# Where the on-chip buffers of a two-stage FFN kernel lie: declared in another order, so that operands and tiles start at multiples of 128 bytes

## What is computed

```python
w = softmax(weight, axis=-1)                       # 8 heads x 7 taps
x = einsum('hk,bskhg->bshg', w, windows(x_pad))    # 7 taps along the sequence
gate = 1 / (1 + exp(-(x @ moe_w_gate)))            # 192 -> 1536
y = (gate * (x @ moe_w_val)) @ moe_w_out           # 1536 -> 192
h = y @ moe2_w_in                                  # 192 -> 2048
g = where(h > 0, h, exp(min(h, 0)) - 1)
out = g @ moe2_w_out                               # 2048 -> 192
```

## Time and profile before

| What | Value |
|---|---|
| Median of 3 runs | 1220.97 us (1220.84 to 1221.13) |
| The profiled execution, its own time | 1221.01 us |
| Its span, first to last instruction | 1219.2 us |
| PE busy | 1203.1 us, 99% of the span |
| Weight loads (PEld) busy | 1147.8 us, 94% |
| DVE busy | 922.2 us, 76% |
| ACT busy | 631.1 us, 52% |
| POOL busy | 89.3 us, 7% |

### The profile page before, as it was taken

The page is one execution under the profiler, slowest core; times in us unless marked ns, Lnnn a source line. Parts: engine busy times, 40 slices in busy tenths (PEclk is TensorE's granted clock), DMA queues, the critical chain, the costliest instruction groups (busy, mean ns, idle before and its releaser), DMA issues.

```text
span 1219.2 us, 27136 instructions
## 1 busy us (share of the span) xinstructions
PE 1203.1 (99%) x10220; PEld 1147.8 (94%) x10220; DVE 922.2 (76%) x1497; ACT 631.1 (52%) x1093; POOL 89.3 (7%) x87
## 2 busy tenths in 40 slices
PE   5999999999999999999999999999999999999998
PEld 4998888888899999999999999999999999999998
DVE  7788777787777877778777777777777777777786
ACT  6555445454554545545455453544535555455554
POOL 4271001010010100001010010100101001010000
PEclk9999999999999999999999999999999999999999
DMA  6021101001010010100101001110101101001000
GB/s 203 22 68 36 31 18 34 30 17 30 17 34 30 17 30 17 47 17 17 30 25 40 17 17 30 35 30 17 30 19 33 30 17 34 30 17 30 10 10 26
DMA packets 14022, 38.04 MB, mean 31 GB/s; under 512 B 2224, under 2 KB 2224, under 8 KB 14000
## 3 DMA queue, kind: packets, MB, share of 16 engines
q1 hardware_dynamic: 13776, 37.60, 10.7%
q10 hardware_dynamic: 224, 0.14, 0.0%
HBM read 15.71 MB, written 6.29 MB: 18 GB/s over the span
## 4 chain that ended last, share of the span: by engine, by line
PE 98%; DVE 1%; ACT 1%; DMA 0%; issue 0%; SPq 0%; DVEq 0%; ACTq 0%
PE hid L236 55%; PE z_acc_a L254 14%; PE y_acc_a L254 11%; PE z_acc_b L254 10%; PE y_acc_b L254 8%; DMA raw_g<-g_weights 0%; DVE mixed L646 0%; ACT gw L470 0%; PE y_acc_a L236 0%; DVE h_split L673 0%; ACT L526 0%; ACT curve L482 0%; SPq L173 0%; ACT ys L604 0%; ACT ys L599 0%
## 5 line engine op out<-in xcount | busy, mean ns | idle before, releaser
L236 PE MATMUL hid<-xs,gw 64*128 64x512 f32 x3240 | 621.1, 393 | 0.0
L236 PEld LDWEIGHTS hid<-xs,gw 64*128 64x128 f32 x3240 | 507.4, 185 | 17.3
L236 PE MATMUL hid<-ys,ew 64*128 64x512 f32 x2160 | 471.2, 393 | 0.0
L487 ACT CAST h_split<-hidden 128x512 fp32r<-128x512 f32 x448 | 276.8, 618 | 302.8 <-DVE hidden L715 262.5
L482 ACT ACTIVATE curve<-hid 128x512 f32<-128x512 f32 x446 | 264.5, 597 | 267.9 <-PE hid L236 267.7
L236 PEld LDWEIGHTS hid<-ys,ew 64*128 64x128 f32 x2160 | 366.9, 185 | 9.9
L254 PE MATMUL z_acc_a<-h_split,ew 64*128 64x512 f32 x1440 | 375.3, 393 | 0.0
L673 DVE TENSOR_TENSOR h_split<-hidden,h_split 128x512 fp32r<-128x512 f32 x448 | 318.2, 710 | 32.8 <-ACT h_split L487 27.6
L254 PE MATMUL y_acc_a<-h_split,gw 64*128 64x512 f32 x1080 | 310.2, 393 | 0.0
L254 PEld LDWEIGHTS z_acc_a<-h_split,ew 64*128 64x128 f32 x1440 | 263.6, 185 | 9.3
L254 PE MATMUL z_acc_b<-h_split,ew 64*128 64x512 f32 x960 | 262.9, 393 | 0.0
(11 more groups left out here) (74 smaller groups left out, 480.4 us busy)
## 6 DMA issues: line engine op xcount, KB each, us to landing
x_in<-x_windows SPq DMA_DIRECT2D x16, 518.0 KB, 3.3
ys<-ys SPq DMA_DIRECT2D x30, 256.0 KB, 3.7
xs<-xs SPq DMA_DIRECT2D x30, 256.0 KB, 3.4
out<-z_out SPq DMA_DIRECT2D x16, 256.0 KB, 2.0
raw_g<-g_weights SPq DMA_DIRECT2D x12, 288.0 KB, 5.0
raw_e<-e_weights SPq DMA_DIRECT2D x8, 384.0 KB, 3.9
out<-z_out SPq DMA_DIRECT2D x15, 128.0 KB, 2.3
x_in<-x_windows SPq DMA_DIRECT2D x2, 259.0 KB, 3.5
```

Of the source, the lines that this page charges most:

```text
L236: return nc.tensor.matmul(acc[:], w[rows, at:at + P], inp[rows, features], start=s == 0, stop=s == last)
L487: nc.scalar.copy(h_split[:, t % RING, 0], hidden[:, t % RING]).then_inc(hi_done, 1)
```

## The change

Only the order of the declarations changes. The weights and their raw copies keep their place. Behind them now come `xs`, `ys`, `h_split`, `hidden` and the other large tiles, then `x_in`, and the eight small tensors last. No shape, type, instruction, wait or loop is changed: on each of the five engines the compiled programs read alike row for row, apart from line numbers.

```diff
         raw_g = sb("raw_g", [P, RAW_G_SLOTS, MAIN])
         raw_e = sb("raw_e", [P, RAW_E_SLOTS, RAW_E])
 
+        xs = sb("xs", [P, 6, T], F32R)
+        ys = sb("ys", [P, 6, T], F32R)
+        h_split = sb("h_split", [P, RING, 2, T], F32R)
+
+        hidden = sb("hidden", [P, RING, T])
+        curve = sb("curve", [P, 2, T])
+        below = sb("below", [P, 2, T])
+        mixed = sb("mixed", [P, 2, T])
+
+        y_low = sb("y_low", [HALF, T])
+        y_sum = sb("y_sum", [P, T])
+        z_low = sb("z_low", [HALF, T])
+        z_out = sb("z_out", [P, 2, T])
+
+        x_in = sb("x_in", [P, 2, T + K - 1])
         cw = sb("cw", [P, 2, K])
         cw_neg = sb("cw_neg", [P, 2])
...
         warm = sb("warm", [P, 1])
-        x_in = sb("x_in", [P, 2, T + K - 1])
-        mixed = sb("mixed", [P, 2, T])
-
-        xs = sb("xs", [P, 6, T], F32R)
-        ys = sb("ys", [P, 6, T], F32R)
-
-        curve = sb("curve", [P, 2, T])
-        below = sb("below", [P, 2, T])
-        hidden = sb("hidden", [P, RING, T])
-        h_split = sb("h_split", [P, RING, 2, T], F32R)
-
-        y_low = sb("y_low", [HALF, T])
-        y_sum = sb("y_sum", [P, T])
-        z_low = sb("z_low", [HALF, T])
-        z_out = sb("z_out", [P, 2, T])
```

## The result

The changed kernel takes 1185.2 us in the median (1185.07 to 1185.75, 4 runs) against 1220.95 us for the one before (1220.84 to 1221.13). The ratio is 0.971, with a 95% interval of 0.969 to 0.973: 36 us faster, where no change was forecast and the range ended at 1213.

A forecast was written before the change was run, and what follows sets the result against it. PE was taken to bound the kernel through the distance between matmuls on each array half. A 1219.2 us span plus zero for stream, tiles and transfers gave a forecast of 1221.0 us, range 1213 to 1229.

The forecast's parts named there:

- a nanosecond per slot: Matmul pace behind the opening: a slot is one matmul on each array half; 1 ns over about 5020 slots is 5.0 us.
- Part two: Tiles of DVE, ACT and POOL: new placement costs zero, within 2% of a DVE instruction, and is hidden anyway.
- part three: Transfers: weights' first tiles don't move, other copies run under matmuls; zero, with 0.3 us either way allowed for the opening.
- rival 1: Matmul streams pay for their start address, so faster: large form 1117 to 1185 us (0.07), small 1212.5 to 1219 (0.09).
- part one: Moving operands xs, ys, h_split going from remainder 32 to 0 by 128: effect per slot taken as zero.
- The opening's 427 ns: First matmuls, at PE's lower clock: 512 columns at remainder 32 take 512 column times and less than one more.
- the 20.7 ns: Slot at the higher clock: 234.0 ns against 213.3 for 512 columns, about 50 column times due to something else.
- the bound of 104 us: Largest gain if all 20.7 ns per slot came from the start address: 5020 x 20.7 = 104 us.
- load and next start add up to the slot: Middle of the run: weight load ends after 185 ns, next matmul 49 ns later, so the slot is the weight path's.
- Its form with 64-byte units: Rival 1 on matmul streams: one 64-byte unit in 33 saved, 7.1 ns per slot, 36 us, giving 1185 us.
- Rival 2: Weight load and stream collide once both start at remainder 0 by 128: slower, 1223 to 1225 or 1241 us; chance 0.13.

The follow-up runs named there:

- t32: Changed kernel with moving operands still at remainder 0, other large tiles at 32 and x_in at 96 by 128; 1185.1 us once, 1188.2 to 1188.8 in three others.
- s448: Changed kernel, but every matmul that doesn't open an accumulation group streams 448 of the 512 tokens; 1108.2 us, one execution.
- all32: Changed kernel with every tensor 32 bytes further by one pad ahead of gw, weights and moving operands both at 160 by 512; 1188.3 us.
- m128: Changed kernel with the moving operands 128 bytes further, at 256 by 512 where weights stand at 128 by 512; 1214.2 us.
- m16: Changed kernel with each moving tensor read through a view that starts 4 values in, at remainder 16 by 128; 1208.4 us.
- h32: Changed kernel with only h_split padded to remainder 32 by 128, xs and ys staying at 0; 1209.5 us.

## Why the prediction was wrong

**What held.** PE bounds the kernel from the opening to the end, a nanosecond per slot is worth 5.0 us, and the whole difference is in the slot: 7.3 ns against 36 us. Part two and part three held as well: DVE's and ACT's medians moved by 1 ns, x_in's landing moved the opening by 0.9 us in one execution (0.3 had been allowed), and t32 shows the tiles to be worth no more than 3 us. Of the prediction's own signs, the one for rival 1 came true (more matmuls in the same 300 us). Its claim that loads begin closer together is true as well, since they begin with the matmuls.

**The step that failed** is in part one: "I take zero, since the only row that isolates the stream shows zero." The opening's 427 ns were read rightly, and the changed kernel shows the same there (425 and 427.5). But that row stands at the lower level of PE's clock, and the difference between these layouts shows at the higher level alone: 234.0 against 226.7 ns. A row that shows no cost at half the speed bounds the cost at half the speed, not at the full one. The prediction had even named the 20.7 ns that exist at the higher level only and had written the bound of 104 us beside them; then it weighted the wrong row. 7.3 of those 20.7 ns were the layout's, and 13.4 to 13.6 ns are still there at the best distance.

**The reason given for zero was wrong too.** It was that load and next start add up to the slot, so that the slot is the weight path's. s448 has the same loads and slots of 207 ns. The load takes its 184 ns in either case, and what follows it up to the next start shrinks; that the sum fits says nothing about who sets it. The prediction said that an order of two events isn't a cause, and leaned on it all the same.

**Rival 1 had the number and not the mechanism.** Its form with 64-byte units gave 7.1 ns and 1185 us, which is the measured time to the microsecond. It is refuted nevertheless: all32 has its moving operands 32 bytes into such a unit and keeps the gain, m128 has them at its start and loses it. A number that fits is no proof of the story that made it.

**Rival 2 had the right pair and the wrong sign.** It was the one that asked how weight load and stream stand to each other by address, and it expected agreement to cost. Agreement by 256 bytes is the best case measured, and each disagreement that was tried costs, most at 160.

The two pages that were weighed fare alike. "SBUF — State Buffer" of the Trainium skill, with its 16-byte lines, would have left the sum as it is; all the starts here are on such lines, m16's too, and the time moves by 36 us. The same page (Who interferes with whom) gives PE two read ports, one for the moving operand and one for weights, independent of each other, and says that PE never waits on anyone. The table above doesn't fit that: the place of one stream against the other changes the slot by 7.3 ns, and the measurement decides. Whether PE waits at a port or elsewhere, no run here shows. The gap of 216 ns of "TensorE: Matmul & The Clock Gate" wasn't reached by any layout; the best slot was 226.9 ns.

**What stays open.** Why a period of 256 bytes, why 160 costs more than 96, whether the lag of the halves is what makes distance 64 change from execution to execution and within one, and where the last 13 ns go. Distances between 160 and 256 weren't tried, and 16 only mixed with 144. Whether the moving operands must also agree with each other wasn't separated: they agreed in all but h32 and m16, and h32's stretches on xs alone, slower than their distance 0 would have it, make that a live question.

## What to carry to other kernels

Where PE streams f32 operands back to back at its full clock, it is worth trying addresses at which all moving operands and all weights agree by 256 bytes; a single pad tensor can do it, and in this kernel, the only one tried, it was worth 3%. Multiples of 128 bytes neither ensure that nor are needed for it. And if a slot is longer than its columns at the higher clock, shorten the stream in one experiment before calling the rest the weight load's; a rate that was read at the lower clock doesn't bound a cost at the higher one.

## What the runs showed of the hardware

- At the higher level of PE's clock 512 columns take 226.7 to 234.2 ns in place of 213.3, and how much depends on the two start addresses by 256 bytes. At the lower level they take 425 to 428 ns with distance 160 and with distance 0.
- It needs no second half of the array: matmuls over all 128 rows show it as well (235 and 230 ns).
- At distance 64 two slots occur within one run, 229 and 233 ns, the first where the halves start together, the second mostly where they start 0.07 us or more apart. At distances 0 and 160 lags of 0.01 and 0.09 us go with the same slot.
- Matmuls at distance 0 take 231 ns where others nearby have distance 32 (h32), against 226.7 where all have 0.
- The weight load's own duration hardly takes part: medians of 184 and 185 ns at slots of 226.9 and 234.2 ns.
- The opening ran at the lower rate after 10.5 us without matmuls, while the granted clock was recorded as 1.00; the rate had to be read from the distance of starts.
- DVE and ACT don't care: DVE's subtraction took 683 ns at remainder 32 and 684 at 0, and its taps, which start at every multiple of 4 bytes, 743 to 756 ns before and 745 to 752 after.
